# First MLP products ahead of the test for unlikely expert tiles; block 1's rows turned by DMA transfers

## The reference, cut to what matters

```python
# 1. retention attention: 4 batches, 8 heads, 768 steps, head size 64 -> x (3072 x 512)
# 2. mixture of experts, 8 experts, each token goes to its argmax expert
for e in range(8):
    mask = e_idx == e
    h = np.maximum(x[mask] @ w1[e], 0.0)           # 512 -> 1024
    out[mask] = gate_w[mask, None] * eom[mask, e, None] * (h @ w2[e])
# 3. gated MLP on the 3072 rows
rms = np.sqrt(np.mean(x * x, axis=-1, keepdims=True) + 1e-06)
xn = x / rms * rms_g
g = xn @ w_gate                                    # 512 -> 1536
silu = g * (1.0 / (1.0 + np.exp(-g)))
val = xn @ w_val
return silu * val @ w_out                          # 1536 -> 512
```

## Time and profile before

| what | us |
|---|---|
| median of 3 runs | 1109.93 |
| the runs | 1109.93, 1109.16, 1111.65 |
| the profiled execution, its own time | 1112.05 |
| span of its trace (first to last instruction) | 1110.3 |
| TensorE busy in the span | 1093.7 |

### The profile page before, as it was taken

One profiled execution on the slowest core, in us unless ns is written; L12 is line 12 of the kernel. 1 busy time (PEld: TensorE's weight loads), 2 busy tenths in 40 slices (PEclk: granted clock), 3 DMA queues, 4 the chain that ended last, 5 costly groups with the idle time before them and its releaser, 6 DMA issues.

```text
span 1110.3 us, 20452 instructions
## 1 busy us (share of the span) xinstructions
PE 1093.7 (99%) x6307; PEld 910.1 (82%) x6308; DVE 442.6 (40%) x886; ACT 378.5 (34%) x619; POOL 176.8 (16%) x245
## 2 busy tenths in 40 slices
PE   6999999999999999999999999999999999999998
PEld 6888888888888888887888888888888888888887
DVE  4777767333424325431443332423333243243222
ACT  2544435343525446432223331232133122212112
POOL 2444423322221200100001300110030011001000
PEclk9999999999999999999999999999999999999999
DMA  9999825433444533422201200011020001101001
GB/s 216 233 259 238 247 69 197 163 112 116 123 121 157 186 123 115 158 84 91 76 1 38 76 20 19 29 47 38 0 76 19 19 18 57 38 0 38 1 1 39
DMA packets 114069, 101.53 MB, mean 91 GB/s; under 512 B 81856, under 2 KB 87392, under 8 KB 114016
## 3 DMA queue, kind: packets, MB, share of 16 engines
q1 hardware_dynamic: 98752, 66.07, 22.1%
q0 software_dynamic: 8832, 26.81, 7.5%
q10 hardware_dynamic: 6432, 7.96, 2.0%
HBM read 76.41 MB, written 20.22 MB: 87 GB/s over the span
## 4 chain that ended last, share of the span: by engine, by line
PE 96%; DVE 2%; issue 1%; DMA 0%; ACT 0%; POOL 0%; SPq 0%; POOLq 0%; DVEq 0%
PE banks L654 15%; PE bank L730 15%; PE bank L731 15%; PE bank L732 15%; PE bank L627 14%; PE banks L730 3%; PE banks L731 3%; PE banks L732 3%; PE bank L538 2%; PE banks L524 2%; PE bank L568 2%; PE banks L642 1%; PE bank L618 1%; PE bank L576 1%; PE bank L642 1%; PE banks L517 1%
## 5 line engine op out<-in xcount | busy, mean ns | idle before, releaser
L1409 DVE TENSOR_TENSOR gated<-bank,sig 128x512 f32<-128x512 f32 (+1 forms) x78 | 50.7, 650 | 341.8 <-ACT sig L1022 341.8
L1022 ACT ACTIVATE sig<-bank 128x512 f32<-128x512 f32 x72 | 43.1, 598 | 327.2 <-PE bank L732 327.1
L730 PE MATMUL bank<-xh,w1h 128*128 128x512 f32 x384 | 149.6, 390 | 0.0
L731 PE MATMUL bank<-xl,w1h 128*128 128x512 f32 x384 | 149.6, 390 | 0.0
L732 PE MATMUL bank<-xh,w1l 128*128 128x512 f32 x384 | 149.6, 390 | 0.0
L730 PEld LDWEIGHTS bank<-xh,w1h 128*128 128x128 f32 x384 | 72.1, 188 | 15.0
L732 PEld LDWEIGHTS bank<-xh,w1l 128*128 128x128 f32 x384 | 72.1, 188 | 14.9
L731 PEld LDWEIGHTS bank<-xl,w1h 128*128 128x128 f32 x384 | 72.1, 188 | 14.8
L1031 ACT ACTIVATE hh<-prod 128x512 fp32r<-128x512 f32 (+1 forms) x78 | 46.7, 599 | 109.9 <-DVE prod L1417 108.9
L1176 DVE TENSOR_TENSOR hidl<-bank,hidh 128x512 fp32r<-128x512 f32 x29 | 20.1, 692 | 130.4 <-ACT hidh L881 130.4
L1423 DVE TENSOR_TENSOR hl<-prod,hh 128x512 fp32r<-128x512 f32 (+1 forms) x78 | 50.9, 652 | 51.2 <-ACT hh L1031 51.2
(11 more groups left out here) (243 smaller groups left out, 2144.5 us busy)
## 6 DMA issues: line engine op xcount, KB each, us to landing
stage<-in_moe_w SPq DMA_DIRECT2D x64, 512.0 KB, 5.6
expert_rows<-tile_o ACTq DMA_DIRECT2D x29, 256.0 KB
q_raw<-in_q SPq DMA_DIRECT2D x24, 256.0 KB, 5.7
k_raw<-in_k SPq DMA_DIRECT2D x24, 256.0 KB, 6.0
v_raw<-in_v SPq DMA_DIRECT2D x24, 256.0 KB, 4.4
stage<-stage SPq DMA_DIRECT2D x64, 64.0 KB, 2.0
stage<-in_moe_w_out SPq DMA_DIRECT2D x6, 512.0 KB, 4.1
stage<-in_moe_w_gate SPq DMA_DIRECT2D x5, 512.0 KB, 6.8
```

Source lines behind the costliest of these rows:

```text
L730: pe.matmul(out_ap, lh, rh, start=first, stop=False)
L731: pe.matmul(out_ap, lh, rl, start=False, stop=False)
L1022: nc.scalar.activation(sig[:], bank[GV[f % 2][0]][:, :], ACT.Sigmoid).then_inc(s["sig_done"], 1)
L1409: v3.tensor_tensor(gated[:, part], bank[GV[f % 2][0]][:, part], sig[:, part], ALU.mult)\
```

## The change

1. `gate_part` is the inner product of `gate_value`, given a name. `first_gate_value` computes the gate product of step 0 of block 0 and three quarters of the value product. It stands ahead of the `If` on `unlikely`, and a second copy of it stands at the end of the `If`'s body, behind the loop over tiles 27 to 32. The last quarter of the value product follows behind the `If`. `ffn_block(0)` leaves gate_value(0, 0) out. `skip_group_check` is an argument for the simulator.
2. Block 1 is turned by transfers as blocks 2 to 5 are; its TensorE transposes are gone.
3. In block 0, steps 0 to 3 split two pieces each; steps 4 to 7 none.
4. The rows of the next block: in block 0 the mean square and the scaling of the rows both come at step 7 (before: 9 and 10), the scale factors are staged at step 6 (before: 8). In the other blocks the mean square moves from step 3 to step 4, where the scaling stays, and the DVE block transposes from step 9 to step 10.

```diff
         def by_transfer(n):
-            return not isinstance(n, int) or n > 1
+            return not isinstance(n, int) or n > 0
...
+        def rows_at(n):
+            return 7 if isinstance(n, int) and n == 0 else 4
...
-            for n in range(2, NBLK):
+            for n in range(1, NBLK):
                 regroup(n)
...
             with pe.Fori(SURE, LIKELY) as a:
                 tile_if_real(a)
-            with pe.If(unlikely):
-                with pe.Fori(LIKELY, TILES) as a:
-                    tile_if_real(a)
...
+            def gate_part(n, f, m, i, stop_at=KD - 1):
+                return three(bank[GV[f % 2][m]][:, :], gate_parts(m, f, i), (xh[:, i, :], xl[:, i, :]),
+                             i == 0, i >= stop_at)
+
+            def first_gate_value():
+
+                pe.wait_ge(s["early_done"], 2)
+                pe.wait_ge(s["xl_ready"], KD)
+                for i in range(KD):
+                    gate_part(0, 0, 0, i)
+                for i in range(KD - 1):
+                    gate_part(0, 0, 1, i, KD - 2)
+
+            first_gate_value()
+            with pe.If(unlikely):
+                with pe.Fori(LIKELY, TILES) as a:
+                    tile_if_real(a)
+                first_gate_value()
+            gate_part(0, 0, 1, KD - 1).then_inc(s["gv_done"], 1)
...
             def ffn_block(n):
-                turns = not by_transfer(n + 1)
                 for f in range(NF):
-                    gate_value(n, f)
-                    if f == NF - 1 and turns:
-                        pe.wait_ge(s["prod_done"], step_no(n, NF - 1))
-                        turn_xn(n + 1, [0])
+                    if f or not isinstance(n, int) or n:
+                        gate_value(n, f)
                     if f:
                         down(n, f - 1)
-                if turns:
-                    pe.wait_ge(s["prod_done"], step_no(n + 1, 0))
-                    turn_xn(n + 1, [1])
                 down(n, NF - 1)
...
-                    if isinstance(n, int) and n == 0 and f < RUN:
-                        split_rest(f)
-                    if f == (3 if by_transfer(n + 1) else NF - 3) and not final:
+                    if isinstance(n, int) and n == 0 and f < RUN // 2:
+                        split_rest(2 * f)
+                        split_rest(2 * f + 1)
+                    if f == rows_at(n) and not final:
                         norm_stats(n + 1)
...
-                    if f == (2 if by_transfer(n + 1) else NF - 4):
+                    if f == rows_at(n) - 1:
                         stage_scale(n + 1)
-                    if f == (4 if by_transfer(n + 1) else NF - 2):
+                    if f == rows_at(n):
                         normalise(n + 1)
-                    if f == NF - 3 and by_transfer(n + 1):
+                    if f == NF - 2:
                         turn_grouped(n + 1)
```

More of the change, by code:

```diff
@@ L339, in head_of, with turned_bank @@
             return 4 * c + 2 * a + r
-        def turned_bank(n, kd):
-            return bank[FREE[kd % 2]] if isinstance(n, int) and n == 0 else bank[GV[kd // 2][kd % 2]]
+        def turned_bank(kd):
+            return bank[FREE[kd % 2]]
         def turned(n, kd):
-            return split_rows[:, kd, :] if by_transfer(n) else turned_bank(n, kd)[:, :]
+            return split_rows[:, kd, :] if by_transfer(n) else turned_bank(kd)[:, :]
+        def rows_at(n):
+            return 7 if isinstance(n, int) and n == 0 else 4
         def halves(f):
@@ L691, in _, with turn_first @@
                 down_tile(a, 0)
-            def turn_xn(n, halves):
+            def turn_first(half):
                 for t in range(BLK):
[L695 to L702, removed]
+                    pe.wait_ge(s["norm_done"], t + 1)
+                    for i in range(2):
+                        kd = 2 * half + i
+                        mm = pe.transpose(turned_bank(kd)[:, t * P:(t + 1) * P],
+                                          block_rows(0, t)[:, kd * P:(kd + 1) * P], ident)
+                        if t == BLK - 1:
+                            mm.then_inc(s["xn_turned"], 1)
             pe.wait_ge(s["control_ready"], 1)
@@ L709, in _ @@
             extra = pe.value_load(flags[0:1, 2:3], min_val=0, max_val=TILES - SURE)
-            turn_xn(0, [0])
+            turn_first(0)
             unlikely = pe.value_load(real[0:1, LIKELY:LIKELY + 1], min_val=0, max_val=1)
@@ L713, in _ @@
             pe.wait_ge(s["xl_ready"], 2)
-            turn_xn(0, [1])
+            turn_first(1)
             def tile_if_real(a):
@@ L721, in _ @@
                 tile_if_real(a)
-            with pe.If(unlikely):
-                with pe.Fori(LIKELY, TILES) as a:
-                    tile_if_real(a)
             def three(out_ap, lhs, rhs, first, last):
                 (lh, ll), (rh, rl) = lhs, rhs
-                pe.matmul(out_ap, lh, rh, start=first, stop=False)
-                pe.matmul(out_ap, lh, rl, start=False, stop=False)
-                return pe.matmul(out_ap, ll, rh, start=False, stop=last)
+                pe.matmul(out_ap, lh, rh, start=first, stop=False, skip_group_check=True)
+                pe.matmul(out_ap, lh, rl, start=False, stop=False, skip_group_check=True)
+                return pe.matmul(out_ap, ll, rh, start=False, stop=last, skip_group_check=True)
             def weights_ready(n, m, f):
@@ L751, in gate_value @@
                             pe.wait_ge(s["xl_ready"], KD * n + i + 1)
-                        mm = three(bank[GV[f % 2][m]][:, :], gate_parts(m, f, i),
-                                   (xh[:, i, :], xl[:, i, :]), i == 0, i == KD - 1)
+                        mm = gate_part(n, f, m, i)
                 mm.then_inc(s["gv_done"], 1)
@@ L967, in turned_hi @@
                 if by_transfer(n):
-                    act.wait_ge(s["grouped_turned"], KD * GROUPS * (n - 2) + GROUPS * (kd + 1))
+                    act.wait_ge(s["grouped_turned"], KD * GROUPS * (n - 1) + GROUPS * (kd + 1))
                 else:
-                    act.wait_ge(s["xn_turned"], KD * n + kd + 1)
+                    act.wait_ge(s["xn_turned"], kd + 1)
                 if isinstance(n, int) and n == 0:
@@ L1357, in turn_grouped @@
             def turn_grouped(n):
-                dve.wait_ge(s["regrouped"], 16 * GROUPS * GROUPS * (n - 1))
+                dve.wait_ge(s["regrouped"], 16 * GROUPS * GROUPS * n)
                 for kd in range(KD):
```

## The result

The changed kernel's median is 1113.69 us (7 runs, 1113.03 to 1114.49), before's 1109.81 (7 runs). The ratio is 1.0032, 95% interval 1.0022 to 1.0042, so between 2.4 and 4.7 us. Forecast were +2.9 us and 1112.9. The profiled execution took 1114.20 us, against a forecast of 1115.0.

The account below looks back on a forecast made before the run. TensorE was taken to bound the kernel, busy 1093.7 us of a 1110.3 us span. The terms +4.76 - 1.78 - 0.05 = +2.93 us took the median from 1109.93 to 1112.9 us, range 1110.6 to 1115.2.

Parts of the forecast that it names:

- The test is true: At the If before the MLP: 29 real tiles, so tiles 27 and 28 run inside it and both product copies execute.
- 21 more matmuls, +4.76: TensorE at about 488 us, ahead of the If: 21 added matmuls at 0.2267 us each, nothing hiding them, +4.76 us.
- The stop stays, less one jump: TensorE before the MLP: the 2.04 us idle stretch, four skipped tests, stays; one covered jump saves 0.05 us.
- Rival B: At the If: the test is false in timed runs, one copy covers the idle stretch; -5.6 us, 1104.4 us, chance 0.03.
- The transposes, -1.78: TensorE at the end of block 0: block 1's sixteen transposes go, 7.52 us becoming 5.74, -1.78 us.
- Nothing late on the other engines: DVE, ACT and SP in the MLP blocks: new transfers, block transposes, scaling and paired splits stay under cover, cost 0.
- The clock, "left in at the same size: 0": Block 0's first 24 matmuls, behind the idle stretch: the 1.73 us lost to the lower clock stays, change 0.
- the sum moves both alike: Whole program: the +2.93 us shifts the profiled execution (1112.05) and the median (1109.93) equally, giving 1115.0 and 1112.9.
- Rival A: Behind the idle stretch: the clock keeps its level, 1.73 us come back; +1.2 us, 1111.1 us, chance 0.16.
- C: At the door of the If: a jump waits to fetch its code; up to +4.9 us, 1114.9 us, chance 0.08.
- D: At gate_value(1, 0): block 1's rows come late and TensorE waits for xl; say +2, 1114.9 us, chance 0.04.

Follow-up runs that it names:

- both_test29: The changed kernel with LIKELY = SURE + 5, so the test is false and the products run once: 1105.71 us, ratio 0.9961 against before.
- two_skips: The kernel before with TensorE's second loop ended two tiles earlier, so two skipped tests are made and not four: 1107.60 us, ratio 0.9976.
- before_test29: The kernel before with only LIKELY = SURE + 5, so tiles 27 and 28 join the first loop and the test is false: 1107.49 us, ratio 0.9975.
- transfers_only: The changed kernel with the first products back behind the If only; block 1 by transfers and two-piece splits stay: 1107.90 us, ratio 0.9982 against before.
- one_piece: both_test29 with one weight piece split a step in block 0 (steps 0 to 7): 1116.05 us, ratio 1.0048 against before.
- products_only: The kernel before with only the 21 first MLP products ahead of the test and again inside the If: 1116.01 us, ratio 1.0055.
- early_21: The kernel before with 21 unused matmuls added ahead of tile 2, far ahead of the stop: 1113.76 us, ratio 1.0034.
- gate_only: The kernel before with only the gate product's 12 matmuls ahead of the test and again in the If: 1113.94 us, ratio 1.0028.

## Why the prediction was right

**The test is true.** It was: 29 tiles, two copies, both in the trace. Everything else in the forecast's sign hangs on this count; with the test false, both_test29 shows what the change gives.

**21 more matmuls, +4.76.** 4.76 us in the trace of the changed kernel. At equal clocks the five variants that ran extra matmuls near the test or far from it cost 2.9 to 3.2 for 12, 4.0 to 5.4 for 21 and 8.5 to 9.7 for 42.

**The stop stays, less one jump.** 2.03 against 2.04 us. The jump taken out of it, put at 0.05, can't be seen. That the stop is the skipped tests was argued by elimination; two_skips and before_test29 showed it. Rival B priced the stop at its 2.04 us of idle time, where taking it away gave 2.2.

**The transposes, -1.78.** 1.69 in the trace, 1.8 in transfers_only. The stretch from the start of step 11's last gate product to block 1 is 618.96 - 613.14 = 5.82 us, and not the 5.74 of the boundary from block 1 to 2. The trace has a weight load of down(0, 11) that stands 0.28 us for DVE's low part (616.10), as its like at the other boundary does for 0.22 (711.93). Before, eight of the transposes stood there and covered it.

**Nothing late on the other engines.** Step 7's root came at T + 7.9 (7.6 predicted), the scaling ended at T + 10.1 (9.7), the next gate product began at T + 10.0 (9.7). The transfers took 10.1 us to issue (11.3). All of it is under cover, as said, but for the weight load just named. one_piece shows that this cover depends on the pairs, which the prediction priced by themselves at 0 and did not tie to the rows.

**The clock, "left in at the same size: 0".** This is the term that was mis-sized. The prediction took the one profiled execution of before, where the clock fell, as the rule. Before's executions at half speed are 18 of 60, so its median has no fall in it. The step "the sum moves both alike" set the profiled execution, with the fall, and the median, without it, to move together; that held only if equally many executions fell in both kernels, while 6 of 7 executions of the changed kernel have one. That adds up to 1.7 us to the difference of medians. At equal clocks the change costs 1113.84 - 1111.39 = +2.45 us (6 executions at 0.998) and 1113.03 - 1109.68 = +3.35 (one at 1.000), on both sides of the +2.93. The medians, which take in the change in how often the clock falls, differ by +3.9. That the clock term came out unequal and the forecast still held is in part luck: it could have moved the medians by up to 1.7 us, and moved them by about 1. Rival A had the mechanism, that some executions are free of the loss, but put it on the wrong kernel: it was before that was mostly free.

**Rival B** fell with the count of tiles, **C** and **D** with the traces: no other wait at the test, none for block 1's rows.

## What to carry to other kernels

Before judging a branch by its name, count in the trace how often its body ran: here a count of 232 rows said that "unlikely" was the case at hand, and turned 21 matmuls of cover into 21 matmuls of double work. Work put ahead of a test so as to hide the test's cost must not be destroyed by the branch that is taken; where the inputs allow it, as here, moving the bound of the test is worth more (before_test29, -2.4 us, against +6.1 for products_only). Matmuls added as a probe cost their full price only where the engine has no idle time: early_21 filled a gap of 0.6 us. A term "unchanged on both sides" has to be checked over many executions, not in one profile.

## What the hardware did that I had not expected

- A stop of TensorE of about 2 us was enough for the granted clock to go to its 1.2 GHz level for some 3 us, in 44 of the 111 executions that had such a stop. Full-speed and half-speed executions of one kernel differ by 1.7 us. The fall does not come at a fixed distance from the stop: the first matmul at half speed starts 0.4 us after the stop's end in gate_only, 0.8 in before and 1.5 in the changed kernel.
- A skipped test on TensorE's list, with its load of `real[a]`, takes at least 1.0 us if the four take the same. Two of them vanish behind the queued matmuls of the tile before; four do not.
